# Pooled attention results brought to their four queries by the matmuls that add them to the local results

## The reference, cut to what matters

```python
q_d, k_d, v_d = (a.reshape(B, H, 144, 4, D).mean(axis=3) for a in (q, k, v))
out_up = np.repeat(softmax(scale * q_d @ k_d.T) @ v_d, 4, axis=2)
mask = np.abs(pos[:, None] - pos[None, :]) < 4
out_local = softmax(np.where(mask, scale * q @ k.T, -1e9)) @ v
x = rows_of_tokens(out_up + out_local)          # 2304 x 512
x = (h * sigmoid(h)) @ w_out,  h = x @ w_in      # 512 -> 2048 -> 512
x = the same with sigmoid(1.702 * h) and its own weights
```

## Time and profile before

| | |
|---|---|
| median of 3 runs | 809.66 us (809.51 to 809.9) |
| the profiled execution's own time | 809.12 us |
| its span, first to last instruction | 807.3 us |
| TensorE (PE) busy | 789.9 us, 98% of the span |
| VectorE (DVE) busy | 649.1 us, 80% |
| ScalarE (ACT) busy | 530.7 us, 66% |
| GpSimd (POOL) busy | 196.0 us, 24% |
| granted TensorE clock | 1.000 over the core |

### The profile page before, as it was taken

One profiled execution on the slowest core, in us unless ns is written; L12 is line 12 of the kernel. 1 busy time (PEld: TensorE's weight loads), 2 busy tenths in 40 slices (PEclk: granted clock), 3 DMA queues, 4 the chain that ended last, 5 costly groups with the idle time before them and its releaser, 6 DMA issues.

```text
span 807.3 us, 15757 instructions
## 1 busy us (share of the span) xinstructions
PE 789.9 (98%) x5864; PEld 763.4 (95%) x5864; DVE 649.1 (80%) x911; ACT 530.7 (66%) x849; POOL 196.0 (24%) x197
## 2 busy tenths in 40 slices
PE   9888799999999999999999999999999999999998
PEld 5666599999999999999999999999999999999998
DVE  7999899999998778999678898899565688456466
ACT  5878865677655677565687556678455786465673
POOL 5889987520144320246100000000000000000000
PEclk9999999999999999999999999999999999999999
DMA  8777647887777887588877778868887777877773
GB/s 286 260 245 244 194 150 261 274 285 233 251 263 244 279 301 256 197 286 255 288 267 249 239 252 256 263 220 274 300 283 259 275 247 264 300 252 269 267 258 134
DMA packets 100763, 205.51 MB, mean 255 GB/s; under 512 B 8784, under 2 KB 56400, under 8 KB 100688
## 3 DMA queue, kind: packets, MB, share of 16 engines
q1 hardware_dynamic: 100688, 204.51, 76.0%
HBM read 160.96 MB, written 43.52 MB: 253 GB/s over the span
## 4 chain that ended last, share of the span: by engine, by line
PE 78%; POOL 8%; DVE 7%; issue 4%; DMA 1%; ACT 1%; SPq 0%; POOLq 0%; DVEq 0%; ACTq 0%
PE hid L330 41%; PE yp L356 35%; DVE gr L547 2%; POOL vpair L1015 2%; DVE wh L302 2%; POOL vavg L1019 1%; POOL pband L1009 1%; PE yp L372 1%; POOL G L1039 1%; POOL G L1040 1%; DVE xs L257 1%; DMA wr<-sums_out 1%; POOL G L1045 1%; POOL G L1043 1%; POOL x L271 0%
## 5 line engine op out<-in xcount | busy, mean ns | idle before, releaser
L330 PE MATMUL hid<-xs,wh 128*128 128x384 f32 x2016 | 351.2, 334 | 1.3 <-DVE hw L516 0.9
L330 PEld LDWEIGHTS hid<-xs,wh 128*128 128x128 f32 x2016 | 349.3, 188 | 2.3 <-issue 2.0
L356 PE MATMUL yp<-gr,wh 128*128 128x384 f32 x1968 | 342.4, 334 | 0.0
L356 PEld LDWEIGHTS yp<-gr,wh 128*128 128x128 f32 x1968 | 341.1, 188 | 0.3 <-issue 0.3
L293 ACT ACTIVATE wh<-wr 128x1024 fp32r<-128x1024 f32 (+1 forms) x164 | 164.6, 1004 | 151.3 <-PE hid L330 119.0
L547 DVE TENSOR_TENSOR gr<-G,gr 128x768 fp32r<-128x768 f32 x144 | 138.2, 967 | 52.6 <-ACT gr L428 52.6
L428 ACT ACTIVATE gr<-G 128x768 fp32r<-128x768 f32 x144 | 121.9, 846 | 67.3 <-PE yp L356 67.3
L302 DVE TENSOR_TENSOR wh<-wr,wh 128x1024 fp32r<-128x1024 f32 x76 | 91.5, 1203 | 16.5 <-ACT wh L293 16.4
L391 ACT ACTIVATE G<-G 128x1152 f32<-128x1152 f32 x48 | 55.8, 1162 | 0.0
L511 DVE TENSOR_TENSOR hv<-p,hid 128x384 f32<-128x384 f32 x48 | 26.4, 549 | 30.6 <-PE hid L330 26.5
L537 DVE TENSOR_TENSOR G<-hv,hid 128x384 f32<-128x384 f32 x48 | 26.4, 550 | 27.0 <-PE hid L330 26.9
(11 more groups left out here) (98 smaller groups left out, 762.6 us busy)
## 6 DMA issues: line engine op xcount, KB each, us to landing
wh<-rests SPq DMA_DIRECT2D x72, 512.0 KB, 3.7
wr<-sums_out SPq DMA_DIRECT2D x48, 512.0 KB, 4.8
wr<-in_w_out SPq DMA_DIRECT2D x36, 512.0 KB, 5.4
rests<-wh SPq DMA_DIRECT2D x36, 512.0 KB, 3.4
wr<-sums_in SPq DMA_DIRECT2D x40, 384.0 KB, 4.0
wr<-in_w_in SPq DMA_DIRECT2D x40, 256.0 KB, 3.6
qk<-in_qkT SPq DMA_DIRECT2D x11, 576.0 KB, 5.0
G<-in_w_in SPq DMA_DIRECT2D x12, 512.0 KB, 5.1
```

What stands on the lines that cost most here:

```text
L330: last = eng.matmul(hid[:, at, 0:HALF], lhsT=wh[:, w % SLOTS, part, a % 4, cc * P:(cc + 1) * P], rhs=xs[:, rest, q, cc, :], start=start an ...
L356: last = eng.matmul(yp[:, at + m, 0:HALF], lhsT=wh[:, w % SLOTS, part, p % 4, m * P:(m + 1) * P], rhs=gr[:, p, rest, :], start=start and p ...
```

## The change

Four things:

1. TensorE's order becomes `band_scores(u)`, all four groups of transposes of `old`, `avg_scores(u)`, `band_product(old)`, `avg_product(old)`. ScalarE's four copies of the transposes likewise come first in its body.
2. `avg_product` is 8 matmuls of 288 columns in place of 4 of 144. Each pooled column is read four times (a broadcast operand), and the result is added in PSUM on top of the local one. The pooled copies (L1062) write only the 288 columns that are used, divide by four, and sort them by head.
3. ScalarE's copy of the pooled result (`oavg`) and VectorE's addition (L1176) go away. One copy of 576 columns from `po` to `x` takes their place: on VectorE in the bodies of TAKEN, on ScalarE in the others, where it comes before `early` and `normalise`. Both wait for `avg_out`.
4. The tiles are cut a little differently (56, six of 58, two of 57, one of 58 queries), so that no tile crosses the middle of `po`.

```diff
-    FIRST_Q = S - (NT - 1) * NQ
-    q0 = [max(0, FIRST_Q + NQ * (t - 1)) for t in range(NT)]
-    nq = [FIRST_Q] + [NQ] * (NT - 1)
+    nq = [NQ - 2] + 6 * [NQ] + 2 * [NQ - 1] + [NQ]
+    q0 = [sum(nq[:t]) for t in range(NT)]
...
+    TAKEN = (3, 5, 7, 9, 11, 13, 15, 16)
...
-            pta = sb("pta", [P, 2, NA * AR])
+            pta = sb("pta", [P, 2, 2, NA, AQ])
...
+        def results(u):
+            at = (2 * (u.half % 2) + u.odd) * T + (u.half // 2) * S
+            return x[:].rearrange("p c n -> p (c n)")[:, bass.ds(at, S)]
...
@@ block.scalar @@
-                    eng.activation(pta[:, j - NLG, :], src[:, 0:NA * AR], ACT.Copy).then_inc(p_cp, 1)
+                    eng.activation(pta[:, j - NLG].rearrange("p h c q -> p c h q"), by_head(src), ACT.Copy,
+                                   scale=1.0 / FACTOR).then_inc(p_cp, 1)
...
                 if not first:
-                    for j in range(NLG):
+                    for j in range(NG):
                         group(old, j)
...
-                if not first:
-                    for j in range(NLG, NG):
-                        group(old, j)
...
-                if not first:
+                if not first and u.n not in TAKEN:
                     eng.wait_ge(avg_out, old.n + 1)
-                    eng.wait_ge(x_done, 1 + old.n)
-                    eng.activation(oavg, po[:, OA:OA + SD], ACT.Copy,
-                                   scale=1.0 / FACTOR).then_inc(oavg_cp, 1)
+                    eng.activation(results(old), po[:, PO:PO + S], ACT.Copy).then_inc(x_done, 1)
...
@@ block.vector @@
-                if not first:
-
+                if u.n in TAKEN:
                     old = u.before()
-                    eng.wait_ge(oavg_cp, 1 + old.n + 1)
-                    eng.wait_ge(band_out, old.n + 1)
...
-                    eng.tensor_tensor(dst.rearrange("p (s r) -> p s r", r=FACTOR),
-                                      po[:, PO:PO + S].rearrange("p (s r) -> p s r", r=FACTOR),
-                                      oavg.unsqueeze(2).broadcast_to([P, SD, FACTOR]),
-                                      ALU.add).then_inc(x_done, 1)
+                    eng.wait_ge(avg_out, old.n + 1)
+                    eng.tensor_copy(results(old), po[:, PO:PO + S]).then_inc(x_done, 1)
...
@@ block.tensor @@
-                eng.wait_ge(oavg_cp, 1 + u.n)
...
-                                              start=True, stop=True)
+                                              start=t in (1, 5), stop=False, skip_group_check=True)
...
-                for h in range(2):
-                    for j in range(2):
-                        last = eng.matmul(po[h * D:(h + 1) * D, OA:OA + SD], lhsT=vavg[u.odd][:, j, h * D:(h + 1) * D],
-                                          rhs=pta[:, j, :].rearrange("p (c q) -> p c q", c=NA)[:, :, h * QT:h * QT + AQ],
-                                          start=(j == 0), stop=(j == 1))
+                for j in range(2):
+                    for half in range(2):
+                        for h in range(2):
+                            rhs = pta[:, j, h].rearrange("p c q -> p (c q)")[:, half * SD // 2:(half + 1) * SD // 2]
+                            last = eng.matmul(po[h * D:(h + 1) * D, PO + half * S // 2:PO + (half + 1) * S // 2],
+                                              lhsT=vavg[u.odd][:, j, h * D:(h + 1) * D],
+                                              rhs=rhs.unsqueeze(2).broadcast_to([P, SD // 2, FACTOR]),
+                                              start=False, stop=j == 1, skip_group_check=True)
...
-                    for j in range(NLG):
+                    for j in range(NG):
                         group(old, j)
                 if last is not None:
                     avg_scores(u)
...
-                    for j in range(NLG, NG):
-                        group(old, j)
                     band_product(old)
                     avg_product(old)
```

More of the change, by code:

```diff
@@ L817, in build @@
     assert DM == 512 and QT == D == P // 2 and starts[1] > 0 and q0[-1] - starts[-1] == 2 * (FACTOR - 1)
+    assert sum(nq) == S and q0[HALF] == S // 2
     assert all(a + WIN >= min(q + n + FACTOR - 1, S) for a, q, n in zip(starts, q0, nq))
@@ L867, in build @@
             sma = sb("sma", [AR, NA, 2])
-            spare = ffn.spare(HALF * P + SD)
-            ptb, oavg = spare[:, 0:HALF * P].rearrange("p (t n) -> p t n", t=HALF), spare[:, HALF * P:]
-            pta = sb("pta", [P, 2, NA * AR])
+            ptb = ffn.spare(HALF * P).rearrange("p (t n) -> p t n", t=HALF)
+            pta = sb("pta", [P, 2, 2, NA, AQ])
             sc = ps("sc", [P, 2, 512])
@@ L902, in build @@
         band_out, avg_out = sem("band_out"), sem("avg_out")
[L903 removed]
+        x_done = sem("x_done")
         ffn.programs(keep, lambda name, shape: whole.enter_context(nc.psum_tensor(name, shape, F32)))
         block = whole.enter_context(nc.Block())
+        def results(u):
+            at = (2 * (u.half % 2) + u.odd) * T + (u.half // 2) * S
+            return x[:].rearrange("p c n -> p (c n)")[:, bass.ds(at, S)]
         def iterations(eng, start, body):
@@ L1061, in group, with by_head @@
                 else:
-                    eng.activation(pta[:, j - NLG, :], src[:, 0:NA * AR], ACT.Copy).then_inc(p_cp, 1)
+                    eng.activation(pta[:, j - NLG].rearrange("p h c q -> p c h q"), by_head(src), ACT.Copy,
+                                   scale=1.0 / FACTOR).then_inc(p_cp, 1)
+            def by_head(src):
+                from_h = src[:, 0:NA * AR].rearrange("p (c q) -> p c q", c=NA)
+                return bass.AP(from_h.tensor, from_h.offset, [from_h.ap[0], [AR, NA], [QT, 2], [1, AQ]])
             def body(u, first, last):
@@ L1168, in body @@
                     eng.reciprocal(rca[:], rca[:]).then_inc(a_rcp, 1)
-                if not first:
+                if u.n in TAKEN:
                     old = u.before()
-                    eng.wait_ge(oavg_cp, 1 + old.n + 1)
-                    eng.wait_ge(band_out, old.n + 1)
-                    at = (2 * (old.half % 2) + old.odd) * T + (old.half // 2) * S
-                    dst = x[:].rearrange("p c n -> p (c n)")[:, bass.ds(at, S)]
-                    eng.tensor_tensor(dst.rearrange("p (s r) -> p s r", r=FACTOR),
-                                      po[:, PO:PO + S].rearrange("p (s r) -> p s r", r=FACTOR),
-                                      oavg.unsqueeze(2).broadcast_to([P, SD, FACTOR]),
-                                      ALU.add).then_inc(x_done, 1)
+                    eng.wait_ge(avg_out, old.n + 1)
+                    eng.tensor_copy(results(old), po[:, PO:PO + S]).then_inc(x_done, 1)
             def early(n):
@@ L1354 @@
     pairs = v.reshape(B, H // 2, 2, S, D).transpose(0, 1, 3, 2, 4).reshape(B * H // 2, S, 2 * D)
-    starts = [0] + [51 + 58 * t for t in range(8)] + [S - 64]
+    starts = [0, 53, 111, 169, 227, 285, 343, 401, 458, 512]
     windows = np.concatenate([np.stack([pairs[:, a:a + 64] for a in starts[i:i + 5]], axis=2) for i in (0, 5)],
```

2 lines of the change are left out of this document (removed).

## The result

| | before | after |
|---|---|---|
| median | 809.75 us (809.51 to 809.9, 4 runs) | 821.75 us (820.99 to 821.91, 4 runs) |
| span of the profiled execution | 807.3 us | 820.1 us |
| TensorE resumes the unbroken L330 | 106.82 us | 119.57 us |

The changed kernel is slower, by a ratio of 1.0149 (95% interval 1.0136 to 1.0161), 12.0 us. 820.0 was predicted. Where the time went can be read off the last row: TensorE resumes 12.75 us later, and the feed-forward stage behind that moment is as long as it was, 820.1 - 119.57 = 700.5 us against 807.3 - 106.82 = 700.5 us. The granted clock is 1.000 again.

The account below looks back on a forecast made before the run. VectorE, later GpSimd, bound the attention stage. TensorE's 5.09 + 1.46 - 0.2 = 6.35 us units, and ring units up to 7.0, were to resume feed-forward at 117.6 instead of 106.82: 809.12 + 10.8 = 819.9, so 820; range 813 to 825.

Parts of the forecast that it names:

- the ring: Closed wait loop per unit: pooled transposes, `avg_scores`, VectorE's maxima to inversion, ScalarE's scaling, transposes again; 6.75 us, or 5.88 without L257.
- What bounds the kernel: Before the change, TensorE in the attention stage had about 0.9 us slack per unit; VectorE and later GpSimd set the pace.
- Part 1: On TensorE, the wide `avg_product` goes from 0.52 to 1.96 us, rounded to +1.46 us per unit.
- Part 2: On TensorE, two fewer changes of matmul shape save 0.2 us per unit, bounds 0 and 0.3; its unit becomes 6.35 us.
- Part 3: The new order closes the ring: 6.75 us in units 4 and 6, 7.0 in 8; without `early` TensorE's 6.35 rules.
- Part 4: Shared copy on ScalarE 0.63 us, VectorE at most 0.74; ScalarE's waits hidden; units 10, 12, 14 take 7.0.
- The sum: TensorE resumes feed-forward at 117.6 us: first pooled transposes 12.93, 14 steps 92.3, last step 8.6, end 3.8; +10.8 us.
- Heads one after the other: Rival: the wide product's two heads run serially on TensorE, its unit 8.3 us and the time about 848; chance 0.02.
- mild form: Rival: no shape saving, product steps 0.26, ScalarE's queue holding TensorE 0.3 us more; 823 to 827; over 823 0.13, serial included.
- Faster: Rival: product adds under 0.4 us, ring stays open, units 4 and 6 gain about 0.7; 807.5 to 808.5; chance 0.05.
- no change: Rival: TensorE's slack and GpSimd's 6.28 us absorb a product costing 0.9 or less; within 1 us of 809.66; chance 0.05.
- Only the new ring binds: Rival: product adds 0.7 us, TensorE's unit 5.6, so the ring rules every unit; +4.7 us, 814; chance 0.13.

Follow-up runs that it names:

- late remainders: Changed kernel with VectorE's early work (L257, L302) moved from between `mxa` and `smb` to behind the pooled inversion: 819.72 us.
- narrow product: Changed kernel with each of the 8 product matmuls at 72 columns instead of 288, three quarters of the pooled result left out: 820.18 us.
- late remainders and the narrow product: Changed kernel with both edits: early work behind the pooled inversion, and product matmuls of 72 columns: 815.20 us.
- short first group: Changed kernel with late remainders, and the local transposes grouped 2 and 3 instead of 3 and 2: 817.44 us.
- order alone: Kernel before with all four groups of transposes ahead of `avg_scores` on TensorE and ahead of the exponentials on ScalarE, nothing else: 817.94 us.
- old order with the narrow product: Changed kernel with the order of before on TensorE and ScalarE, and product matmuls of 72 columns: 809.15 us.

## Why the prediction was right, and where it was off

The time, the direction and both mechanisms held: TensorE's own unit in some units, the ring in the others. Step by step:

**What bounds the kernel** held, but the slack of 0.9 us was an average: in unit 1 it was 0.24. The time moved as the resume moved, in the changed kernel and in nearly every experiment.

**Part 1** held in mechanism and size: 2.09 us for the product, +1.44 against +1.46 predicted. Eight steps of 288 columns in 2.09 us are 0.26 each with the change of shape in them, against 0.245. The Trainium skill ("TensorE: Matmul & The Clock Gate", section Back-to-back issue gap) would have a step grow by about 19 ns for the 144 more columns, an estimate from its two figures; the trace shows 0.13 growing to about 0.25, so the rows were the better guide here. The rival built on it, that only the ring binds, is out for the changed kernel: the odd units show TensorE without a break.

**Part 2** was too small as a saving and lacked a term. TensorE's blocks need 6.28 us a unit where they follow a wait (39.31 to 45.59), that is 5.09 + 1.44 - 0.25, so the order saves 0.25 us, not 0.2; that it does so by the changes of shape was not tested apart. But the wait for the buffer of the first local group, +0.22 to +0.24, was not seen: 6.52 where TensorE comes unbroken. The wait falls in seven of the 14 steps, 1.7 us in all. Only two of the plain ones are among them; the other five at 6.28 are shorter than the 6.35 predicted, and the two errors nearly cancel, which is luck. The eight of them took 51.7 us, predicted 50.8, and 0.9 of that is one gap, the next point.

**The gap in unit 11** was not predicted and is not explained. From 79.98 to 87.21 is 7.23 us, with TensorE waiting ahead of the pooled transposes:

```profile
85.66 0.77 PE L1205 MATMUL pt<-ident,pband 128*128 128x128 f32 x5
87.21 0.51 PE L1205 MATMUL hp<-ident,pavg 112*128 112x112 f32 x3 [0.78 <-ACT yt L1064]
```

ScalarE had scaled by 85.84, and by the program these transposes wait for nothing later; the copy that the profile names is not theirs to wait for. The same gap of 0.7 us stands in the same unit with late remainders, with the narrow product and with the copies on ScalarE (smaller, 0.23, with late remainders and the narrow product), and is absent with the short first group, with all copies on VectorE and in the order alone. No run isolated it.

**Part 3** held in mechanism; the term was sized too small. Units 4 and 6 took 7.11 us each, not 6.75; unit 8 took 7.49, not 7.0; units 10, 12 and 14 took 7.23, 7.03 and 7.23, not 7.0. Taken from 32.20 to 39.31: both pooled groups 1.03 us (predicted 0.72, and the buffer's wait is in it), `avg_scores` to the maxima 0.92 (0.99), VectorE to the end of the inversion 3.97 (3.86), scaling and hand-overs 1.19 (1.18). The ring without the buffer's wait is what the order alone shows, 6.87; with it 7.11. In units 8, 10 and 14 the early work itself was longer too: L302 took 1.33 us and L257 1.07, where 1.20 and 0.95 were assumed. Seen over the six units, this is +1.7 us.

**Part 4** held. The old order with the narrow product costs nothing that shows, so there the copies and the tile cut are free; in the new order no run takes them out alone. Where ScalarE's queue is what ends last, in unit 12, the step took 7.03 against the 7.0 predicted (its terms, 6.1 + 1.0, make 7.1). The copy took ScalarE 0.65 us (predicted 0.63) and VectorE 0.73 (at most 0.74). ScalarE's wait for the product is hidden, but only just: with the copies on ScalarE in the odd units it is not.

**The sum.** Predicted 12.93 + 92.3 + 8.6 + 3.8 = 117.6. Measured 12.86 + 94.9 + 8.0 + 3.8 = 119.6. The 14 steps carry the miss of +2.6 (ring +1.7, unit 11 +0.9), and the last step gives 0.5 back: the terms for it add up to 8.5 (the sum has 8.6), and 0.4 of that was an idle time ahead of L330 that is gone. That the first start met 12.93 so closely is luck: over the traces with the new order it lies between 12.56 and 14.06. Against before that is +12.75 instead of +10.8, inside the range. The expected signs were there too: GpSimd waited for `rcb` in all 16 units, 29.7 us together, and VectorE waited 15 times for `avg_scores`, 14.9 us; in the kernel before these were 8 waits, 12.5 us, and 6 waits, 2.5 us.

**The rivals.** *Heads one after the other* is out (the product would have taken 4 us). Its mild form, another wait on top, is the nearest to what happened, and covers most of the 2 us: the wait was for a copy in ScalarE's queue, as that rival said, though for a reason it did not name. *Faster* and *no change* rested on a cheap product; the narrow product in the old order is the same as before within its interval, as *no change* would have it, and no run was faster. *Only the new ring binds* is the order alone, and that costs 8.1 us, not the 4.7 of the rival: its steps are 0.12 longer than predicted, 1.7 us over 14, and the clock takes its part.

## What to carry to other kernels

When work is moved onto an engine with slack, write down its whole unit, and beside it each ring that the new order closes; the slower of the two rules each unit, and they don't add. Check every rotating buffer after a reorder: the block that used to cover its copy may be gone, and such a wait shows only in the distance between starts. And try each part of a change in both orders: here the same reorder costs 8 us on one version and brings 1 to 1.5 on the other. Compare such traces step by step against the same step before, not against an average, and leave out the start, which alone moved by over 1 us between traces.

## What the runs showed of the hardware

- The granted clock of TensorE fell in stretches in the kernels where TensorE waited long: in the narrow product to 0.57 in the 4 us behind a stretch in which it was busy 2.17 of 4, with waits up to 1.7 us in that kernel. Long waits alone don't settle it: at 90 to 94 us of the same trace TensorE was busy 2.18 of 4 and the clock stayed at 1.00, as it did throughout the stage in the kernel before, with a wait of 1.5 us. In the changed kernel, whose longest wait there is 0.8 us, it stayed at 1.00 too.
- In the order alone each of three such stretches made its step 1.06 to 1.29 us longer than the same step at full clock.
- VectorE's plain copy of 128x576 out of PSUM takes 0.73 us, no less than the addition with a broadcast operand that it replaced (0.74). ScalarE does the same copy in 0.65.
